# Attention, routed experts and a dense layer: weights of gate and noise in one transfer, and a bank and buffer of their own for the last transposed probabilities

## The reference, cut to what matters

```python
# 1. attention: q, k, v of (4 batches, 8 heads, 576 positions, 64), fp32
scores = (1 / sqrt(64)) * q @ k.T
mask   = (rel >= 0) & (rel < 64)                 # each query sees itself and the 63 keys before it
attn   = exp(scores - max) / (sum + 1e-9)
x      = (attn @ v)  as rows                     # (2304, 512)
# 2. routed experts: 8 experts, 2 per row
logits = x @ w_gate
noisy  = logits + log1p(exp(x @ w_noise)) * noise
top2   = the two largest of noisy; top2_w = softmax over the two
x      = sum over the two: top2_w * (relu(x @ w1[e]) @ w2[e])      # w1 (8, 512, 1024), w2 (8, 1024, 512)
# 3. dense layer
h      = x @ w_in                                # (512, 2048)
g      = h where h >= 1, 0 where h <= -1, else (h + 1)**2 / 4
out    = g @ w_out                               # (2048, 512)
```

## Time and profile before

| | us |
|---|---|
| median of 3 runs | 1077.67 (1076.57 to 1077.71) |
| profiled execution | 1077.91 |
| its span in the trace | 1076.3 |
| PE busy | 1057.4 (98%) |
| GpSimd (POOL) busy | 393.1 (37%) |
| ScalarE (ACT) busy | 356.3 (33%) |
| VectorE (DVE) busy | 344.9 (32%) |

### The profile page before, as it was taken

The page is one execution under the profiler, slowest core; times in us unless marked ns, Lnnn a source line. Parts: engine busy times, 40 slices in busy tenths (PEclk is TensorE's granted clock), DMA queues, the critical chain, the costliest instruction groups (busy, mean ns, idle before and its releaser), DMA issues.

```text
span 1076.3 us, 17647 instructions
## 1 busy us (share of the span) xinstructions
PE 1057.4 (98%) x5848; PEld 884.3 (82%) x5849; DVE 344.9 (32%) x700; ACT 356.3 (33%) x821; POOL 393.1 (37%) x310
## 2 busy tenths in 40 slices
PE   8999979999999999999999999999999999999998
PEld 6888758888888888888888887988888888888886
DVE  5878841112211122111221112332333232333222
ACT  4678432222222222222222221533344334335333
POOL 6223178785827346280462806830010001100000
PEclk9999999999999999999999999999999999999999
DMA  6676645949733325133241412240011002101001
GB/s 190 175 258 183 219 139 195 331 145 351 245 117 117 117 83 170 39 117 117 79 174 39 149 67 69 88 128 20 20 51 48 20 1 79 40 1 40 1 1 40
DMA packets 50195, 120.09 MB, mean 112 GB/s; under 512 B 7072, under 2 KB 12320, under 8 KB 49632
## 3 DMA queue, kind: packets, MB, share of 16 engines
q0 software_dynamic: 16688, 62.66, 17.8%
q1 hardware_dynamic: 19920, 32.62, 9.7%
q10 hardware_dynamic: 13536, 24.12, 6.5%
HBM read 86.88 MB, written 32.51 MB: 111 GB/s over the span
## 4 chain that ended last, share of the span: by engine, by line
PE 92%; DVE 3%; ACT 2%; DMA 1%; issue 1%; ACTq 0%; POOL 0%; SPq 0%; DVEq 0%; POOLq 0%
PE bank L1492 7%; PE bank L1494 7%; PE bank L1511 7%; PE bank L1509 7%; PE bank L1493 7%; PE bank L1510 7%; PE bank L1557 6%; PE bank L1559 6%; PE bank L1558 6%; PE bank L1550 6%; PE bank L1552 6%; PE bank L1551 6%; PE bank L1517 3%; PE bank L1284 2%; PE bank L1476 2%; PE bank L1310 2%
## 5 line engine op out<-in xcount | busy, mean ns | idle before, releaser
L482 POOL TENSOR_TENSOR Wl<-stage,Wh 128x2048 fp32r<-128x2048 f32 x36 | 165.8, 4605 | 3.0
L1161 DVE COPY y_out<-bank 128x512 f32<-128x512 f32 x42 | 29.1, 692 | 355.2 <-PE bank L1511 355.2
L1492 PE MATMUL bank<-Wh,xT_h 128*128 x336 | 135.4, 403 | 1.4 <-issue 0.9
L1199 DVE SCALAR_TENSOR_TENSOR bank<-bank,square 128x512 f32<-128x512 f32 x72 | 50.4, 700 | 254.8 <-ACT square L837 254.8
L1494 PE MATMUL bank<-Wh,xT_l 128*128 x336 | 131.5, 391 | 0.0
L1511 PE MATMUL bank<-Wh,hT_l 128*128 x336 | 131.1, 390 | 0.0
L1509 PE MATMUL bank<-Wh,hT_h 128*128 x336 | 130.9, 390 | 0.1
L1510 PE MATMUL bank<-Wl,hT_h 128*128 x336 | 130.8, 389 | 0.0
L1493 PE MATMUL bank<-Wl,xT_h 128*128 x336 | 130.8, 389 | 0.0
L808 ACT ACTIVATE hT_h<-bank 128x512 fp32r<-128x512 f32 x84 | 45.8, 596 | 252.3 <-PE bank L1517 252.3
L480 POOL CAST Wh<-stage 128x2048 fp32r<-128x2048 f32 x36 | 68.5, 1903 | 157.2 <-PE bank L1511 155.1
(11 more groups left out here) (236 smaller groups left out, 1741.1 us busy)
## 6 DMA issues: line engine op xcount, KB each, us to landing
stage<-w POOLq DMA_DIRECT2D x32, 1024.0 KB, 5.8
y_sorted<-y_out ACTq DMA_DIRECT2D x42, 256.0 KB, 2.1
x_in<-x_sorted ACTq DMA_DIRECT2D x38, 256.0 KB, 2.8
x_sorted<-gath_b SPq DMA_DIRECT2D x20, 256.0 KB, 4.3
v_ring<-vW SPq DMA_DIRECT2D x36, 128.0 KB, 4.4
x_rows<-x_blk SPq DMA_DIRECT2D x36, 128.0 KB, 3.1
x_sorted<-gath_a SPq DMA_DIRECT2D x18, 256.0 KB, 3.5
k_ring<-kT SPq DMA_DIRECT2D x8, 512.0 KB, 5.7
```

The source lines that it names most:

```text
L482: nc.gpsimd.tensor_tensor(Wl[:, s, cols], stage[:, c % 2], Wh[:, s, cols], ALU.subtract).then_inc(w_ready, 1)
L1492: nc.tensor.matmul(H_ps[a][:], xT_h[:, u, k], high, start=(k == 0), stop=False)
```

## The change

- The weights of gate and noise are laid side by side on the host (`w_gn_rows`, 128 rows of 64 numbers, 256 bytes each) and loaded with one transfer in place of two. `gn_loaded` is waited for at 16.
- ACT no longer does the copy of iteration 35; DVE does it.
- The transposed probabilities of the last head step (35) go to bank 1 (`S_ps[1]`) and to the second half of `q_ring`, in place of `PT_ps` and `probsT`. PE transposes them in iteration 36, directly behind those of head step 34, without a wait for `pT_copied`. DVE's copy of them (iteration 37) waits for `q_spread` in place of `pv_done`.

```diff
-BY_SCALAR = (15, 16, 17, 19, 20, 21, 22, 23, 26, 29, 32, 35)
+BY_SCALAR = (15, 16, 17, 19, 20, 21, 22, 23, 26, 29, 32)
...
+        def probsT_of(s):
+            return q_ring[:, 1].rearrange("p b c -> p (b c)")[:, 0:J * P] if s == G - 1 else probsT[:]
+
+        def PT_of(s):
+            return S_ps[1] if s == G - 1 else PT_ps
...
-            sp.dma_start(w_gn[:, :, 0:E], w_gate.rearrange("(a p) e -> p a e", p=P)).then_inc(gn_loaded, 16)
-            sp.dma_start(w_gn[:, :, E:2 * E], w_noise.rearrange("(a p) e -> p a e", p=P)).then_inc(gn_loaded, 16)
+            sp.dma_start(w_gn[:].rearrange("p a e -> p (a e)"), w_gn_rows).then_inc(gn_loaded, 16)
...
                 if 2 <= s < G + 2 and s not in BY_SCALAR:
                     dve.wait_ge(pT_done, s - 1)
-                    if s >= 3:
+                    if s == G + 1:
+                        dve.wait_ge(q_spread, 2 * B * (BLOCKS - 1))
+                    elif s >= 3:
                         dve.wait_ge(pv_done, s - 2)
-                    nc.vector.tensor_copy(probsT[:], PT_ps[:]).then_inc(pT_copied, 1)
+                    nc.vector.tensor_copy(probsT_of(s - 2), PT_of(s - 2)[:]).then_inc(pT_copied, 1)
...
             def transposed_probs(s):
                 pe.wait_ge(exp_done, s + 1)
-                if s >= 1:
+                if 1 <= s < G - 1:
                     pe.wait_ge(pT_copied, s)
                 for j in range(J):
-                    mm = nc.tensor.transpose(PT_ps[:, P * j:P * j + P], probs[:, s % CH, P * j:P * j + P], ident[:])
+                    mm = nc.tensor.transpose(PT_of(s)[:, P * j:P * j + P], probs[:, s % CH, P * j:P * j + P], ident[:])
...
-                        mm = nc.tensor.matmul(X_ps[s % 2][Q * hi:Q * hi + Q, Q * j:Q * j + Q], probsT[rows, head],
+                        mm = nc.tensor.matmul(X_ps[s % 2][Q * hi:Q * hi + Q, Q * j:Q * j + Q], probsT_of(s)[rows, head],
...
-                    pe.wait_ge(gn_loaded, 32)
+                    pe.wait_ge(gn_loaded, 16)
...
-                if 2 <= s < G + 2:
+                if 2 <= s <= G:
                     transposed_probs(s - 2)
+                if s == G:
+                    transposed_probs(G - 1)
                 if 3 <= s < G + 3:
                     values(s - 3)
```

More of the change, by code:

```diff
@@ L46, in k_slot, with build @@
     return 2 * (r % 2) + r // 2 % 2
-def build(nc, qT, kT, vW, noise, w_gate, w_noise, w1, w2, w_in, w_out, out):
+def build(nc, qT, kT, vW, noise, w_gn_rows, w1, w2, w_in, w_out, out):
     BLOCKS, _, B, JQ = qT.shape
@@ L1651, in by_slot, with by_row @@
         return np.ascontiguousarray(a).reshape(128, -1)
+    def by_row(a):
+        return a.reshape(a.shape[0] // 128, 128, a.shape[1]).transpose(1, 0, 2)
+    gn = np.concatenate([by_row(moe_w_gate), by_row(moe_w_noise)], axis=2)
     vW = np.ascontiguousarray(v.reshape(B, 2, H // 2, S, D).transpose(0, 3, 2, 1, 4)).reshape(B, S, H * D)
     arrays = {
-        "qT": by_partition(q), "kT": by_partition(k), "vW": vW, "noise": by_slot(moe_noise), "w_gate": moe_w_gate,
-        "w_noise": moe_w_noise, "w1": moe_w1, "w2": moe_w2, "w_in": moe2_w_in, "w_out": moe2_w_out,
+        "qT": by_partition(q), "kT": by_partition(k), "vW": vW, "noise": by_slot(moe_noise),
+        "w_gn_rows": np.ascontiguousarray(gn.reshape(128, -1)), "w1": moe_w1, "w2": moe_w2, "w_in": moe2_w_in, "w_out": moe2_w_out,
     }
```

## The result

The changed kernel takes 1082.72 us (median of 8 runs, 1080.82 to 1084.06) against 1077.78 us for the kernel before (8 runs, 1076.57 to 1080.12). The ratio is 1.0034, with a 95% interval of 1.0021 to 1.0047: slower by about a third of a per cent (3.7 us by the ratio, 4.9 us between the medians). The prediction was 1077.8 us with no change as the likeliest case, and its range ended at 1079.2. It was wrong: the time lies above the range.

What follows compares the result with a forecast made beforehand. PE was taken as the bound, busy 1057.4 of 1076.3 us. Terms of -0.2 us at the start and +0.35 at the end gave +0.15 on the median 1077.67, so 1077.8 us; range 1075.8 to 1079.2.

Steps and rivals of the forecast that it cites:

- Part 1, the transfer: Start of attention: merged weight load lets the second query block land sooner; 0.2 us gained, bounds -0.2 to 0.6.
- the landing at 14.52 against 13.9 worked out: Second query block's arrival, change to key block 1: small packets may cost it 0 to 0.6 us; 0.2 taken.
- Part 2, the placing of instructions: Last attention steps, 111 to 122 us: +0.65 for later values of 33, -0.24 for the own buffer; +0.35 us in sum.
- the hand-over: From the copy of 35 to the routing: same chain as today, 5.18 us, so routing starts at 122.2.
- Rival B: First expert tile: later routing makes the clock drop on dense matmuls, costing 1.7 to 2.0 us; 1079.7 to 1080.0; chance 6%.
- the start's drop: Head steps after PE's 2.05 us wait at key block 1: clock falls to 0.50, costing 1.24 + 0.48 = 1.7 us.
- Rival A: Change to key block 1: query block lands 0.5 us sooner, clock holds; 1.85 us gained, 1075.8; chance 14%.

Runs made afterwards that it cites:

- four matmuls of fill: The changed kernel with four throw-away matmuls on PE ahead of the values of head step 35, where PE stands 1.26 us; 1078.91 us, ratio 0.9998.
- copy on ACT: The changed kernel with the copy of iteration 35 returned from DVE to ACT; 1082.65 us, ratio 1.0033.
- fill at the start: The kernel before with six throw-away matmuls on PE ahead of the scores of head step 4; 1078.44 us, ratio 0.9993.
- kernel before again: The kernel before, unchanged and profiled a second time; 1077.76 us in one execution.

## Why the prediction was wrong, point by point

- **Part 1, the transfer.** Right that it is hidden in the time; the gain of 0.2 us can't be told from none. My argument for it, the landing at 14.52 against 13.9 worked out, rested on one execution of a number that goes from 4.3 to 6.4 us over the profiles. The 0.76 us by which the start came later in the profile after are of that size too: there the block was issued 0.68 us later (9.80 against 9.12) and landed after 5.5 us instead of 5.4.
- **Part 2, the placing of instructions.** Right, nearly to the tenth. Exponentials of 35 issue 0.20 us after the bias (0.20 expected). The values of 33 came 0.66 us later relative to the scores of 35 (112.96 - 109.23 = 3.73, and 114.52 - 110.13 = 4.39; expected 0.65). With the four transposes back in their place 0.57 us of this are gone. DVE ran without a wait from the copy of 34 to the last copy, and the last copy came 0.27 us later (expected 0.35 with bounds -0.25 and 0.8). Timeline of DVE of the kernel after, the answer to the earlier trace rows:

```profile
112.57 0.69 DVE L1027 COPY probsT<-bank 128x512 f32<-128x512 f32 x1 [0.23 <-PE bank L1317]
...
115.32 0.69 DVE L1027 COPY probsT<-bank 128x512 f32<-128x512 f32 x1 [0.71 <-PE bank L1317]
...
116.67 0.68 DVE L1008 TENSOR_TENSOR e_xT_l<-bank,e_xT_h 128x512 fp32r<-128x512 f32 x1
117.27 0.68 DVE L911 TENSOR_TENSOR Wl<-stage,Wh 128x512 fp32r<-128x512 f32 x1
117.87 0.68 DVE L1027 COPY q_ring<-bank 128x512 f32<-128x512 f32 x1
```

- **The step that failed is the hand-over.** It said: from the last copy to the routing everything is the same chain as today, 5.18 us. It took 7.57, and the routing started at 125.44, beyond the 122.8 that the prediction named as a sign of being wrong. The term was mis-sized by the clock and not by the order: in the nine profiles whose clock held behind the last copy this step took 5.16 to 5.18 us, 5.17 with the early transposes and four matmuls of fill; in the five with a drop there it took 6.63 to 7.57, and the two shortest of these have the order of before. The step from the routing to the ranks goes the same way, 7.99 to 8.01 us and 9.31 to 10.52. I had noted that the values of 34 on PE come earlier "but nobody on the path asks for them any more", and stopped there. PE getting ahead of DVE is not free: the work that filled its wait was done sooner, the stand of 0.49 us became one of 1.26 us, and PE had the lower clock for the work that came next.
- **Rival B named this mechanism and put it in the wrong place.** It looked for a further drop at the first expert tile, gave it 6%, and priced it at 1.7 us from the start's drop, where little but head steps followed. At the end of attention the logits and most of the early expert's 24 matmuls lie in the half-speed stretch, with the ranks behind them; two waits of the routing end on these, and it costs 2.39 + 1.79 us in this profile. The range ended below that.
- **Rival A** (the clock holds at the start) happens, but less often than the steps suggest. In eight of the twelve experiments' profiles the step behind the first scores of block 1 takes 2.5 us, with either form of the transfer. Only five of these are free of a drop in the first 25 us; in the other three (copy on ACT, fill at the start, kernel before again) it came sooner, from about 11 us on for 3.4 us, behind a stand of 2.1 to 2.8 us ahead of the first block's scores. Over all fourteen profiles a stand of 1.8 to 2.9 us ahead of the scores of block 1 was followed by a drop in six of six, and one of 0.3 to 1.1 us in none of six. That stand mostly goes with the landing of the query block, and so with the count over the two forms of the transfer given above: whether the change has a hand in it is open, and the times don't show it.

## What to carry to other kernels

When a change moves PE's work ahead of another engine's chain, write down PE's idle pieces as well as the path: a stand that costs nothing in the schedule can cost the clock of what follows. Price a drop by the work that lies behind it up to the next wait for PE, not by a drop elsewhere. If a drop comes in some executions and not in others, compare the share of executions that have it, over ten or more, and not one profile with another.

## What the runs showed of the hardware

A stand of 1.26 us, behind a stretch in which PE otherwise worked, was followed by 6.8 to 10.2 us at a granted clock of 0.50, although PE was busy in them without a pause (10.20 of 10.20 us). The clock mean that goes with it is there in 24 of 28 executions of the kernels with that stand, and in 13 of 112 of those with one of 0.5 us. In two profiles with the stand of 0.49 us a drop of 6.8 us followed as well. What decides in the single execution was not settled. A stand of 2.02 us near 109 us was followed by none, where stands of 1.89 and 2.58 us at about that place were followed by 6.8 and 3.4 us at 0.50. Stands of 0.8 us went both ways, by the clock mean in 3, 2 and 1 of 10 executions of three kernels.
